# Three chained layers in fp32 split products on one core: order of ScalarE's and VectorE's work in the second layer and at the change of layer

## The reference

```python
def _attn_ref(q, k, v, tau):                      # q, k, v: 1 x 6016 x 256
    qn = q / (np.linalg.norm(q, axis=1, keepdims=True) + 1e-06)
    kn = k / (np.linalg.norm(k, axis=1, keepdims=True) + 1e-06)
    s = kn.transpose(0, 2, 1) @ qn / tau          # 256 x 256
    a = np.exp(s - s.max(-1, keepdims=True))
    a /= a.sum(-1, keepdims=True) + 1e-09
    return v @ a
def _moe_ref(x, w_in, w_out):                     # 256 -> 2048 -> 256
    h = x @ w_in
    g = np.where(h >= 1, h, np.where(h <= -1, 0.0, (h + 1) ** 2 / 4))
    return g @ w_out
def _moe2_ref(x, w_gate, w_val, w_out, rms_g):    # 256 -> 1536 -> 256
    xn = x / np.sqrt(np.mean(x * x, axis=-1, keepdims=True) + 1e-06) * rms_g
    g = xn @ w_gate
    return g * (1.0 / (1.0 + np.exp(-g))) * (xn @ w_val) @ w_out
```

## Time and profile before

| | before |
|---|---|
| median of 3 runs | 1113.59 us (1112.51 to 1114.6) |
| the profiled execution, its own time | 1116.33 us |
| its span, first to last instruction | 1114.5 us |
| mean granted TensorE clock | 0.997 |
| TensorE matmuls | 1097.2 us busy (98%) |
| TensorE weight loads | 909.1 us busy (82%) |
| VectorE | 872.9 us busy (78%) |
| ScalarE | 798.9 us busy (72%) |
| chain that ended last | TensorE 90%, VectorE 4%, ScalarE 3%, issue 2%, DMA 1% |
| DMA | 48.77 MB, mean 44 GB/s |

### The profile page before, as it was taken

One profiled execution on the slowest core, in us unless ns is written; L12 is line 12 of the kernel. 1 busy time (PEld: TensorE's weight loads), 2 busy tenths in 40 slices (PEclk: granted clock), 3 DMA queues, 4 the chain that ended last, 5 costly groups with the idle time before them and its releaser, 6 DMA issues.

```text
span 1114.5 us, 14343 instructions
## 1 busy us (share of the span) xinstructions
PE 1097.2 (98%) x4970; PEld 909.1 (82%) x4970; DVE 872.9 (78%) x1271; ACT 798.9 (72%) x1149; POOL 2.3 (0%) x13
## 2 busy tenths in 40 slices
PE   8999999999999999999989999999999999999998
PEld 7877878888888888888868788887887887888997
DVE  5878887888888887889978878777877878777665
ACT  4678888898898898888876565567567557456554
POOL 0000000000000000000000000000000000000000
PEclk9999999999999999999999999999999999999999
DMA  9810112002002010022140010111111002011012
GB/s 337 303 30 1 17 41 57 0 20 57 1 33 39 1 39 1 1 70 64 57 127 21 1 39 20 20 36 38 36 20 39 10 11 52 1 20 20 1 19 53
DMA packets 109018, 48.77 MB, mean 44 GB/s; under 512 B 85266, under 2 KB 99218, under 8 KB 108946
## 3 DMA queue, kind: packets, MB, share of 16 engines
q1 hardware_dynamic: 108946, 47.86, 15.6%
HBM read 35.52 MB, written 12.32 MB: 43 GB/s over the span
## 4 chain that ended last, share of the span: by engine, by line
PE 90%; DVE 4%; ACT 3%; issue 2%; DMA 1%; SPq 0%; DVEq 0%; ACTq 0%
PE ps L1218 16%; PE ps L1220 16%; PE ps L1219 16%; PE ps L1236 8%; PE ps L1237 7%; PE ps L1238 7%; PE ps L1257 5%; PE ps L1258 5%; PE ps L1259 5%; PE ps L1293 4%; DVE cv L787 1%; DMA qk_sb<-in_k_dram 1%; PE ps L1188 1%; DVE cg L787 1%; PE ps L1278 1%
## 5 line engine op out<-in xcount | busy, mean ns | idle before, releaser
L430 ACT ACTIVATE s<-ps 128x512 f32<-128x512 f32 (+1 forms) x360 | 209.5, 587 | 35.0 <-PE ps L1220 22.9
L1218 PE MATMUL ps<-xc_hi,wc_hi 128*128 128x512 f32 (+1 forms) x504 | 199.4, 396 | 6.9 <-ACT s L430 3.9
L1219 PE MATMUL ps<-xc_lo,wc_hi 128*128 128x512 f32 (+1 forms) x504 | 194.9, 387 | 0.0
L1220 PE MATMUL ps<-xc_hi,wc_lo 128*128 128x512 f32 (+1 forms) x504 | 194.6, 386 | 0.0
L430 ACT ACTIVATE h_hi<-cg 128x512 fp32r<-128x512 f32 (+1 forms) x144 | 88.9, 618 | 93.3 <-DVE cg L899 89.6
L1236 PE MATMUL ps<-g_hi,wo_hi 128*128 128x512 f32 (+1 forms) x384 | 150.6, 392 | 0.4 <-DVE g_lo L803 0.2
L1237 PE MATMUL ps<-g_lo,wo_hi 128*128 128x512 f32 (+1 forms) x384 | 148.1, 386 | 0.0
L1238 PE MATMUL ps<-g_hi,wo_lo 128*128 128x512 f32 (+1 forms) x384 | 148.0, 385 | 0.0
L787 DVE TENSOR_TENSOR h_sb<-ps,s 128x512 f32<-128x512 f32 (+1 forms) x144 | 97.8, 679 | 59.2 <-PE ps L1220 58.6
L1218 PEld LDWEIGHTS ps<-xc_hi,wc_hi 128*128 128x128 f32 x504 | 94.8, 188 | 35.9 <-DVE cv L787 10.2
L803 DVE TENSOR_TENSOR g_lo<-h_sb,g_hi 128x1024 fp32r<-128x1024 f32 (+1 forms) x96 | 114.8, 1196 | 11.1 <-ACT g_hi L430 10.0
(11 more groups left out here) (130 smaller groups left out, 1867.7 us busy)
## 6 DMA issues: line engine op xcount, KB each, us to landing
qk_sb<-in_q_dram SPq DMA_DIRECT2D x10, 512.0 KB, 9.8
qk_sb<-in_k_dram SPq DMA_DIRECT2D x10, 512.0 KB, 10.3
y_scratch<-y_sb SPq DMA_DIRECT2D x10, 512.0 KB, 3.0
xraw<-y_scratch SPq DMA_DIRECT2D x10, 512.0 KB, 4.2
out_dram<-outT_sb SPq DMA_DIRECT2D x80, 64.0 KB, 1.9
vstage<-in_v_dram SPq DMA_DIRECT2D x64, 64.0 KB, 2.3
wo_raw<-in_moe_w_out_dram SPq DMA_DIRECT2D x7, 512.0 KB, 9.4
w_in_raw<-in_moe_w_in_dram SPq DMA_DIRECT2D x4, 512.0 KB, 12.1
```

What stands on the lines that cost most here:

```text
L430: return nc.scalar.activation(dst, src, ACT.Copy, **kw)
L1218: nc.tensor.matmul(dst, w_h, x_h, start=p in ("p1", "p2", "p7"), stop=False, skip_group_check=True)
L1219: nc.tensor.matmul(dst, w_h, x_l, start=False, stop=False, skip_group_check=True)
L1220: nc.tensor.matmul(dst, w_l, x_h, start=False, stop=True, skip_group_check=True).then_inc(made[p], 1)
```

## The change

Work is moved within the lists of ScalarE and VectorE; no computation is added or dropped, and TensorE's matmuls are the same.

- Step r = 0: xc_high of p5 moves to the end of group 47, that of p3 goes ahead of g_high; on VectorE xc_low of p4 and p5 go ahead of combine11, g_low behind combine22. The leftover pieces are spread 1/1/2 over p6/p4/p5 of both groups. h_high(0, 0, 0) waits for half the leftover pieces only. The second copy_y moves to step r = 1, behind s2. The first copy_y moves behind s1.
- At the first step of a tile copy_out(T-1, 0) moves behind s1 of m = 1.
- In every step but a tile's last, multiply2(r, 0) moves behind combine22 of m = 1; in the next step multiply2(r-1, 1) moves ahead of h_low(r-1, 1, 0).
- Steps 2 to 4: normalising and row spreading are cut into smaller parts and put at other places.
- Phase one, first tile: one of two transposes, and the first xc_sum, move ahead of combine22 of their group.
- `PIECES2` goes from 1/3/4 to 1/2/4.

```diff
-PIECES0 = {(0, "p6"): 1, (0, "p4"): 2, (0, "p5"): 1, (1, "p7"): 1, (1, "p6"): 1, (1, "p4"): 1, (1, "p5"): 1}
+PIECES0 = {"p6": 1, "p4": 1, "p5": 2}
-PIECES2 = {"p6": 1, "p4": 3, "p5": 4}
+PIECES2 = {"p6": 1, "p4": 2, "p5": 4}
...
-                    act.wait_ge(g_used, 2 * N1)
+                    act.wait_ge(g_used, 2 * N1 - 1 + f)
...
                 if into:
                     xc_high(T + 1, "p4")
+                    if last:
+                        xc_high(T + 1, "p5")
...
                 if r == 0:
-                    xc_high(X, "p5")
+                    xc_high(X, "p3")
                     g_high(N1 - 1, 1)
-                    xc_high(X, "p3")
+                if r == 1:
+                    copy_y(WT - 1, 1)
...
+                G += 1
+                spare(s1, "p1", c11_ready, G, n, 1, s1_ready)
                 if onto:
                     copy_out(T - 1, 0)
                 if r == 0:
                     copy_y(WT - 1, 0)
-                G += 1
-                spare(s1, "p1", c11_ready, G, n, 1, s1_ready)
...
-                if r == 0:
-                    copy_y(WT - 1, 1)
...
-            def normalise(i):
+            def normalise_part(i, a):
                 n, where = half(i // 2), inv_place(i)
                 dve.wait_ge(inv_ready, i + 1)
                 dve.wait_ge(xraw_loaded, 32 * (i // 2 + 1))
+                cell = xraw[:, i % 2 + 2 * a, 0:n]
+                nc.vector.scalar_tensor_tensor(cell, cell, rms_gain[:, a:a + 1], inv_rms[where][:, 0:n], ALU.mult,
+                                               ALU.mult).then_inc(x_ready, 1)
+
+            def normalise(i):
                 for a in range(CT):
...
+                    normalise_part(i, a)
...
+                if T == 0 and p in (4, 5):
+                    transpose_v(1, 2 * p - 8)
+                if T == 0 and p == 6:
+                    xc_sum(1, 0)
                 combine(h[:, 2, 0:n], s7, s7_ready, "p5", n1, n, B, c22_ready)
...
                 elif r:
+                    multiply2(r - 1, 1)
                     h_low(r - 1, 1, 0)
-                    multiply2(r - 1, 1)
...
                 else:
+                    xc_low(X, "p4")
+                    xc_low(X, "p5")
                     combine11(cg, r, 0)
-                    xc_low(X, "p4")
                     maximum(N1 - 1, 1)
                     combine21(cg, r, 0)
-                    xc_low(X, "p5")
+                    xc_low(X, "p3")
+                    combine22(cg, r, 0)
                     g_low(N1 - 1, 1)
-                    combine22(cg, r, 0)
-                    xc_low(X, "p3")
...
-                    if j == 3:
-                        normalise(first)
-                        spread_rows(first + 1)
+                    if j in (2, 3):
+                        normalise_part(first, j - 2)
                     if j == 4:
                         wo2_low(2)
-                        normalise(first + 1)
+                        normalise_part(first + 1, 0)
...
-                if not into and r:
+                if T == 0 and j == 3:
+                    spread_rows(first + 1)
+                if T == 0 and j == 4:
+                    normalise_part(first + 1, 1)
+                if not into:
                     h_low(r, 0, 0)
                 combine21(cv, r, 1)
                 if into:
                     xc_low(X + 1, "p7")
-                elif r:
-                    multiply2(r, 0)
...
                 combine22(cv, r, 1)
-                if r == 0:
+                if not into:
                     multiply2(r, 0)
-                    h_low(r, 0, 0)
             r = N2 - 1
+            multiply2(r, 1)
             h_low(r, 1, 0)
-            multiply2(r, 1)
```

More of the change, by code:

```diff
@@ L522, in wc_high @@
                 else:
-                    act.wait_ge(x_ready, 2)
+                    act.wait_ge(x_ready, 2 * CT)
                 s = slice(0, 4) if part == 0 else slice(4, 7)
@@ L769, in xc_sum @@
                 else:
-                    dve.wait_ge(x_ready, 2 * (X - WT + 1))
+                    dve.wait_ge(x_ready, 2 * CT * (X - WT + 1))
                 B11, B12, B21, B22, T1, T2, T4 = (xraw[:, s, 0:n] for s in range(7))
@@ L844, in spread_rows @@
                 if i > 2:
-                    dve.wait_ge(x_ready, i)
+                    dve.wait_ge(x_ready, CT * i)
                 nc.vector.transpose(inv_rms[inv_place(i)][:, 0:n],
                                     invs[:, i, 0:m].unsqueeze(2).to_broadcast([P, m, 32])).then_inc(inv_ready, 1)
-            def normalise(i):
+            def normalise_part(i, a):
                 n, where = half(i // 2), inv_place(i)
@@ L852, in normalise @@
                 dve.wait_ge(xraw_loaded, 32 * (i // 2 + 1))
+                cell = xraw[:, i % 2 + 2 * a, 0:n]
+                nc.vector.scalar_tensor_tensor(cell, cell, rms_gain[:, a:a + 1], inv_rms[where][:, 0:n], ALU.mult,
+                                               ALU.mult).then_inc(x_ready, 1)
+            def normalise(i):
                 for a in range(CT):
-                    cell = xraw[:, i % 2 + 2 * a, 0:n]
-                    last = nc.vector.scalar_tensor_tensor(cell, cell, rms_gain[:, a:a + 1], inv_rms[where][:, 0:n],
-                                                          ALU.mult, ALU.mult)
-                last.then_inc(x_ready, 1)
+                    normalise_part(i, a)
             def wc_sums(j):
@@ L1027, in _ @@
                     if p in (4, 5):
-                        transpose_v(1, 2 * (p - 4))
-                        transpose_v(1, 2 * (p - 4) + 1)
+                        transpose_v(1, 2 * p - 7)
                     if p == 6:
-                        for i in range(4):
+                        for i in range(1, 4):
                             xc_sum(1, i)
@@ L1386, in _ @@
                         if r == 0:
-                            for i in range(done, done + PIECES0.get((m, name), 0)):
+                            for i in range(done, done + PIECES0.get(name, 0)):
                                 piece1(N1 - 1, i)
-                            done += PIECES0.get((m, name), 0)
+                            done += PIECES0.get(name, 0)
                         elif r <= PAIRS2 * (WT - 1):
```

## The result

The changed kernel takes 1098.7 us, the median of 4 runs (1097.41 to 1101.19); the kernel before, beside it, 1114.09 us (4 runs, 1112.51 to 1116.44). The ratio is 0.9867, 95% interval 0.9852 to 0.9882. The profiled execution took 1098.53 us, its span 1096.7 us. A second set of runs of the same kernel gave 1098.72 us and 0.9868 (0.9853 to 0.9883).

A forecast was written before the change was run, and what follows sets the result against it. TensorE was taken to set the time, so only its waits could be won. Terms 2.6 + 3.0 + (1.5 + 2.45 - 0.1 + 1.7) + 1.6 + 2.1 + 1.0, less 0.2, gave 15.7: 1113.6 to 1097.9 us, range 1096.0 to 1102.5.

The forecast's parts named there:

- Idle less 0.15 us: Any wait of the weight loads at 512 columns: it costs its idle time less 0.15 us.
- Part 1: Tiles 1 to 4: multiply2(r, 0) behind combine22 ends 20 waits of p3 at 0.13 us each, 2.6 us.
- rival A: Waits change place as multiply2, h_high and h_low come later; three terms give half, 3.9 us lost: 1101.8 us; chance 0.13.
- Part 2: A tile's first step: s1 ahead of copy_out ends p6's waits, 2.5 us over four tiles, 0.5 in the last: 3.0 us.
- Part 3: Change of layer, steps 0 and 1: four waits cut and the clock fall gone, 1.5 + 2.45 - 0.1 + 1.7 us.
- The fourth wait: Step 1: the 2.62 us wait for s1 ends as ScalarE's first copy runs earlier and copy_y moves; 2.45 us.
- rival B: The clock falls all the same after what is left of the waits: 1.7 us less gain, 1099.6 us; chance 0.08.
- Part 4: Steps 1 to 4: five waits for combine22 of m = 1 shrink, a gain of 1.6 us.
- Part 5: Last tile: five waits for combine22 go through the 1/2/4 split and the moved multiply2, 2.1 us.
- Part 6: Phase one, first tile: transposes and a sum moved into holes cut waits, 1.0 us, bounds 0.3 and 1.35.
- C: Slower: VectorE's list lags 1.3 us, combine22 of m = 0 late in some 29 steps, 1115.3 us; chance 0.04.
- D: Every wait has a second close behind it, so the change does not do what it says: 1113 us; chance 0.03.

The follow-up runs named there:

- the probes above: Changed kernel plus chains of small ScalarE copies ahead of s1 in each of tiles 1 to 4, two kernels differing in copy numbers: 1108.82 and 1109.56 us.
- the one with copy_out moved: Changed kernel with copy_out(T-1, 1) moved behind s2 of the next step and h_low(0, 0, 0) behind combine21: 1097.05 us, 0.9857.
- the one with the old splits: Changed kernel with step 0's splitting of p5 and p3 and g_low in the old order, leftover pieces still 1/1/2: 1099.82 us, 0.9877.
- the second with small copies: Changed kernel plus 9, 12, 5 and 7 small ScalarE copies ahead of s1 in the fifth step of tiles 1 to 4: 1109.56 us.
- the first kernel with small copies: Changed kernel plus 5, 7, 9 and 12 small ScalarE copies ahead of s1 in the fifth step of tiles 1 to 4: 1108.82 us.

## Why the prediction was right, point by point

**What bounds.** TensorE sets the time and only its waits can be won: shown. Loads' busy time is unchanged and the gain is found where the waits were.

**The signs named ahead.** p3 of step 0 was to load 6.6 us behind the start of the step and p6 of step 1 17.0 us behind it (the 563.7 and 574.1 us of the prediction, less the 557.13 us at which step 0 began before); they load 6.63 and 16.95 us behind it. A step of the last tile takes 13.65 us, as forecast, and no wait for `cv` is left in tiles 1 to 4. One sign of being wrong came too: a wait for `s` in m = 0, in the second step of each tile.

**Idle less 0.15 us.** Read from one wait of 0.28 us, it held within 0.1 us for all sizes in the probes above.

**Part 1.** The 20 waits for `cv` went, as forecast, and p3's load follows without idle time. The price of 0.13 us each was right: with the new waits out of the way, the four middle steps of tile 1 went from 60.44 to 59.84 us, 0.15 us a step, a little more. What failed is the sentence "I cost this at nothing for tiles 1 to 4". I had followed the later multiply2 along VectorE only. Its other consumer is h_high(r, 1, 0) on ScalarE, and behind that, at a tile's first step alone, stands copy_out(T-1, 1) of 1.01 us. The price is about 0.25 us in each of tiles 1 to 4, and a wait of 0.3 us in the last. This is rival A's mechanism, "the waits change place", at one place of a size of 1 us, not its 3.9 us. The other half of the move, multiply2(r-1, 1) ahead of h_low, was worth more than I said: about 1.0 us in step 1, which the sum holds under the 2.45 us of part 3.

**Part 2.** 0.78 - 0.15 us for each tile and 0.45 in the last, 3.0 us; undoing it cost 3.1 us. The 0.15 us of cover for s7 was enough: no wait of p4 shows.

**Part 3.** The split order was forecast at 1.5 us and measured at 1.6. For p3 of m = 1 in step 0 I had walked VectorE to a wait of about 0.45 us; it is there, in the changed kernel, with 0.47 us:

```profile
567.83 0.19 PEld L1224 LDWEIGHTS ps<-xc_hi,wc_hi 128*128 128x128 f32 x1 [0.47 <-DVE cv L788]
```

and moving h_low(0, 0, 0) behind combine21 gave back 0.38 us, against the 0.35 us that I said would stay. The fourth wait and the clock were 2.45 + 1.7 us; undoing one line, the copy's condition, cost 2.6 + 1.5 = 4.1 us. Had the clock fallen all the same (rival B), step 1 would have stayed near 16.7 us; it takes 15.08.

**Part 4.** Steps 2 to 5 gained 1.31 us. With steps 0 and 1 the sum of parts 3 and 4 is 7.32 us against 7.15. Most of the 1.31 us is step 3, from 15.87 to 14.96 us; undoing the moves of multiply2 brought back 0.16 us of it. That the rest comes from the smaller parts of normalising and row spreading is argued from their places, as no run put these back.

**Part 5.** 2.1 us were forecast, 1.63 came. Of the two causes named, the split 1/2/4 carries it alone, and multiply2 nothing in the sum. The size was missed mainly because TensorE's own pace differs here, with no wait in sight. Stretch 1045 to 1065 us in the last tile, the changed kernel, then the one with copy_out moved:

```profile
1045.00:1065.00 20.00, 20.00 (x125) 18.90 (x124) 13.95 (x25) 10.96 (x20) 0.00 (x0) 1.00 0.16 27
```

```profile
1045.00:1065.00 20.00, 20.00 (x126) 19.09 (x125) 12.70 (x22) 10.99 (x20) 0.00 (x0) 1.00 0.16 27
```

Three loads of 448 columns take 0.62 us in the one and 0.61 us in the other, and half a step, without a wait, 6.83 us and 6.77 us; the kernel before, the one with the old splits and the second with small copies have the faster pace too. Over the eight halves of steps 31 to 34 that is 0.5 us, the size of the miss (they take 54.77, 54.18 and, with the old splits, 54.39 us); the new wait for `s` in step 31 adds 0.15 us. Both executions of the changed kernel show the slower pace, and so do four of its edits and the first kernel with small copies, which differs from the second in the number of copies alone. In the changed kernel step 30 still has the faster pace. What sets the pace was not tried and stays open.

**Part 6.** 1.0 us forecast (0.3 to 1.35), 1.20 came, and 1.3 when undone.

**The way to the median.** The forecast of 1097.9 us stood on a median of 1113.6 us for the kernel before; beside the changed one it took 1114.1 us. That is 0.5 of the 0.8 us between forecast and result, and 0.3 us are the smaller gain (15.4 against 15.7 us). The clock's term rested on one execution. Over 21 further ones of the kernel before, the mean clock was 0.997 in 3 (1116.2 us on average), 0.998 in 11 (1114.2 us) and 1.000 in 7 (1112.7 us). A fall that costs 1.7 us lowers the mean over 1114 us by 0.0015, so by this estimate the typical run has one fall, some have none, and the profiled one, at 0.997, was of the kind with two. The profile shows both: one fall behind the 2.62 us, at 579 us, and one at 12.6 us, ahead of phase one, behind a wait of 2.90 us for the inputs. The prediction looked at phase two alone; the mean of 0.997 that it quotes stood for two falls. That start is likely a good part of why the profiled execution lay 2.7 us above the median: its part ahead of phase one took 64.32 us, where the shortest of the thirteen took 61.41 us. The 1100.6 us forecast for the profiled execution carried that slow start along, and 1098.53 us came. And a clock of 0.998 does not say which of the two falls it was: eight executions of the changed kernel had 0.998 twice, 0.999 twice and 1.000 four times. So the term of 1.7 us is right for an execution with the fall, and how many had it is not known.

**Luck in the sum.** That 15.7 and 15.3 us lie so close owes something to errors that cancel. The new waits for `s` cost about 1.2 us where 0.2 us were taken off for small new waits, with 1.0 us more as the bound, and part 5 brought 0.5 us less. Against that the waits of part 1 in the middle steps were worth 0.16 us each and not 0.13, parts 3 and 4 brought 0.2 us more, part 6 0.2 us and part 2 0.1 us. The lower end of the range is not quite what its terms give: 1097.9 less 0.35, 0.2 and 1.0 us is 1096.35, not 1096.0 us.

**The rivals.** C, the slower one, asked for a lag of 1.2 us on VectorE; no wait for `cg` shows in tiles 1 to 4. D would have shown the waits of the earlier trace rows under other names, about as long; the waits on an engine over phase two sum to 3.2 us now, where they were 19.0.

## What to carry to other kernels

When an instruction is moved back in a list, follow every reader of its result on every engine to the next thing that TensorE needs, and do it for the odd steps of a tile as well as for the common one: the move of multiply2 was free on VectorE in tiles 1 to 4, and cost 0.25 us on ScalarE in one step of six. Price each wait as its idle time less what the loads run ahead (0.1 to 0.15 us here), and look at the granted clock behind every long wait, here from 2.48 us on, since a fall cost 1.5 to 1.7 us more. Do so over the whole span: the kernel before had its second fall ahead of phase one, where the prediction did not look. Time stages from one fixed instruction to the next: here they repeated within 0.1 us, where whole runs differ by 3 to 4 us.

## What the runs showed of the hardware

- The granted clock fell from 2.4 to 1.2 GHz after idle times of TensorE's loads of 2.48 us (twice of two), 2.59, 2.62 and 2.90 us, 3.07 us (once of two) and 3.50 us (once of two), never after one of up to 2.22 us. In phase two a fall cost 1.5 to 1.7 us. I had not expected that the same wait at the same place of the code would go either way. The Trainium skill, "TensorE: Matmul & The Clock Gate", section "What's actually happening", says that the throttled state is the default and activity releases it; that agrees with falls behind long waits alone. The same section says that the chip's look at the activity runs freely and does not start with the kernel, so that the point of a change of clock varies from run to run. It would fit the two cases of 3.50 us and the two of 3.07 us, but no run here shows where that look stood.
- With operands of 448 columns and no waits, one load followed another every 0.207 us in the changed kernel and every 0.203 us in three others of almost the same code and in the kernel before; in step 30 of the changed kernel, too, it was 0.203 us. At 512 columns no such difference showed: a step without waits took 14.96 to 14.98 us in all of these.
- The part ahead of phase one, in which the inputs are loaded, lasted 61.4 to 64.4 us from one execution to another with the same code. That range is as large as most single edits here are worth.
